# Attention diagonals and gate weights by small matmuls in a three-stage kernel

## The reference, cut to what matters

```
for t in range(S):
    cur = np.einsum('bhd,bhe->bhde', u[None] * kt, vt)
    y[:, :, t] = np.einsum('bhd,bhde->bhe', rt, state + cur)
    state = wt[:, :, :, None] * state + np.einsum('bhd,bhe->bhde', kt, vt)
```

## Time and profile before

| what | value |
|---|---|
| median of 3 runs | 981.27 us (980.72 to 982.27) |
| profiled execution, its own time | 980.96 us |
| its span, first to last instruction | 979.2 us |
| mean granted clock of TensorE | 0.992 |
| busy: PE, weight loads, DVE, ACT, POOL | 97%, 91%, 69%, 54%, 23% |
| first matmul of stage two (L786) | at 93.7 us of the span |

### The profile page before, as it was taken

One profiled execution on the slowest core, in us unless ns is written; L12 is line 12 of the kernel. 1 busy time (PEld: TensorE's weight loads), 2 busy tenths in 40 slices (PEclk: granted clock), 3 DMA queues, 4 the chain that ended last, 5 costly groups with the idle time before them and its releaser, 6 DMA issues.

```text
span 979.2 us, 18038 instructions
## 1 busy us (share of the span) xinstructions
PE 947.8 (97%) x6825; PEld 894.3 (91%) x6825; DVE 676.2 (69%) x1133; ACT 528.0 (54%) x986; POOL 222.8 (23%) x209
## 2 busy tenths in 40 slices
PE   6989999999999999999989999999999999999995
PEld 4656999999999999999989999999999999999995
DVE  6997769888888875437766765757767468565570
ACT  4454445454555544326545665756657467565560
POOL 0000000202020111021453233333243332334321
PEclk9999999999999999999999999999999999999998
DMA  9996343544445121126557887877968779787751
GB/s 346 302 320 184 115 142 116 160 150 129 134 143 163 50 71 38 51 67 234 188 161 191 237 278 233 250 235 220 307 205 247 254 207 292 218 242 256 200 156 17
DMA packets 94347, 183.74 MB, mean 188 GB/s; under 512 B 18274, under 2 KB 49764, under 8 KB 94260
## 3 DMA queue, kind: packets, MB, share of 16 engines
q1 hardware_dynamic: 80884, 161.90, 50.8%
q0 software_dynamic: 12976, 20.66, 10.2%
q10 hardware_dynamic: 400, 0.02, 0.0%
HBM read 156.94 MB, written 26.97 MB: 188 GB/s over the span
## 4 chain that ended last, share of the span: by engine, by line
PE 87%; DVE 5%; ACT 3%; issue 2%; DMA 1%; SPq 0%; another core or an unknown queue 0%; POOL 0%; DVEq 0%; ACTq 0%; POOLq 0%
PE pp L1231 20%; PE bank L1215 20%; PE bank L786 13%; PE bank L803 7%; PE fx L786 6%; PE fx L803 4%; PE yu L1274 3%; PE pp L184 3%; PE tr L1196 2%; PE yu L1256 1%; PE fx L1256 1%; PE yu L205 1%; PE yu L235 1%; PE tr L193 1%; DVE kdiv L263 1%
## 5 line engine op out<-in xcount | busy, mean ns | idle before, releaser
L1125 POOL DMA_INDIRECT result<-x2s,who x55 | 92.5, 1681 | 290.3 <-ACT x2s L1348 277.4
L1335 DVE SCALAR_TENSOR_TENSOR abl<-bank,abh 128x512 fp32r<-128x512 f32 x96 | 66.2, 691 | 113.7 <-ACT abh L1330 97.5
L976 POOL DMA_INDIRECT slot_entry<-entry,slot_i x48 | 52.1, 1086 | 334.7 <-DVE token_f L965 322.5
L1215 PE MATMUL bank<-xh,set_up_h 128*128 128x256 f32 x384 | 109.2, 284 | 0.0
L1215 PE MATMUL bank<-xh,set_up_l 128*128 128x256 f32 x384 | 108.6, 283 | 0.0
L1215 PE MATMUL bank<-xl,set_up_h 128*128 128x256 f32 x384 | 108.6, 283 | 0.0
L1330 ACT ACTIVATE abh<-bank 128x512 fp32r<-128x512 f32 x96 | 57.5, 599 | 85.1 <-PE bank L1215 79.6
L786 PE MATMUL bank<-xh,w12h 128*128 128x384 f32 x264 | 89.5, 339 | 1.0 <-DVE xl L483 0.9
L786 PE MATMUL bank<-xh,w12l 128*128 128x384 f32 x264 | 88.4, 335 | 0.0
L786 PE MATMUL bank<-xl,w12h 128*128 128x384 f32 x264 | 88.2, 334 | 0.0
L1231 PE MATMUL pp<-set_down_h,abh 128*128 128x384 f32 x256 | 87.7, 342 | 0.0
(11 more groups left out here) (254 smaller groups left out, 2641.4 us busy)
## 6 DMA issues: line engine op xcount, KB each, us to landing
up_raw<-in_moe_w SPq DMA_DIRECT2D x93, 512.0 KB
down_raw<-in_moe_w SPq DMA_DIRECT2D x124, 384.0 KB
wt<-in_w SPq DMA_DIRECT2D x16, 384.0 KB, 3.2
kt<-in_k SPq DMA_DIRECT2D x16, 384.0 KB, 3.1
rt<-in_r SPq DMA_DIRECT2D x16, 384.0 KB, 3.6
vs<-in_v_rows SPq DMA_DIRECT2D x16, 384.0 KB, 3.7
kn<-in_k_rows SPq DMA_DIRECT2D x16, 288.0 KB, 3.2
rn<-in_r_rows SPq DMA_DIRECT2D x16, 288.0 KB, 3.6
```

What stands on the lines that cost most here:

```text
L976: nc.gpsimd.indirect_dma_start(slot_entry, bass.IndirectOffsetOnAxis(slot_i[:, s, n:n + 1], 0), entry[:, s, n, :], None).then_inc(scattere ...
L1125: nc.gpsimd.indirect_dma_start(out, bass.IndirectOffsetOnAxis(who[v % 4][:, s, 0:1], 0), yo[v % 2][:, s, 0:DM], None, bounds_check=N - 1, ...
L1215: last = nc.tensor.matmul(bank[m % 2][:, f * T2:(f + 1) * T2], wp[:, kk, c:c + P], xp[:, kk, :], start=(n == 0), stop=(n == 3 * KD - 1))
L1335: nc.vector.scalar_tensor_tensor(hl[:, 2 * m:2 * m + 2, :].rearrange("p a t -> p (a t)"), bank[m % 2][:, :], 0.0, hh[:, 2 * m:2 * m + 2, : ...
```

## The change

For the pairs 0 to 4 (`by_matmul`, g <= 4) the diagonals come another way: one DVE instruction makes k*r*u with dimensions on partitions (`weighed`), six matmuls with a chunk of it as stationary operand and a 128 x 2 matrix of ones and zeros (`heads`) as moving one sum over each head, and ACT copies the 128 x 12 result. The second loads of k and r for these pairs go; `u` is also loaded in turned form (`u_side`), 16 bytes a partition. `ruk` and `added` have one buffer in place of two. A new load of kt or rt now also waits until the weighed product of the pair whose buffer it takes has been made.

The host sends w_out in both orders, so that the transpositions and their copies go and 1.5 MB (`woT`) is loaded in their place. The gates are made by 24 matmuls with blocks of woT as stationary and the 16 gate columns as moving operand. The first block of w3_mm is made without them, in the opening; its 16 columns follow as eight more matmuls (`gates_mm`), once DVE has written the gate columns.

```diff
-          "wo_turn": 2, "wo_gates": 5, "gates_turn": 1, "w3_mm": 5}
+          "wo_gates": 6, "gates_turn": 0, "gates_mm": 3, "w3_mm": 5}
...
+        def by_matmul(g):
+            return g <= HP
...
         def sp_input_load(sp, b, q, n):
             g, i = HP * b + q, q % 2
+            if n and by_matmul(g - 2):
+                need(sp, weighed_ready, g - 1)
...
         def dve_products(dve, b, q, part):
             g, i = HP * b + q, q % 2
-            if part == 0:
+            if by_matmul(g):
+                if part == 0:
+                    for n in (1, 2):
+                        dve.wait_ge(loaded[n][i], 16 * (2 * b + q // 2 + 1))
+                    dve.wait_ge(u_side_loaded, 16)
+                    need(dve, diag_full, g)
+                    nc.vector.scalar_tensor_tensor(weighed[:, :], rt[i][:, :], u_side[:, q:q + 1], kt[i][:, :],
+                                                   ALU.mult, ALU.mult).then_inc(weighed_ready, 1)
...
+        def pe_diag(pe, b, q):
+            g = HP * b + q
+            pe.wait_ge(weighed_ready, g + 1)
+            if g == 0:
+                pe.wait_ge(heads_ready, 4)
+            need(pe, diag_ready, g)
+            for c in range(NC):
+                last = nc.tensor.matmul(bank[0][:, 2 * c:2 * c + 2], weighed[:, c * C:(c + 1) * C], heads[:, :], start=True, stop=True)
+            last.then_inc(diag_full, 1)
...
+        def act_diag(act, b, q):
+            g = HP * b + q
+            act.wait_ge(diag_full, g + 1)
+            nc.scalar.copy(diag[:, :, :].rearrange("p c h -> p (c h)"), bank[0][:, 0:2 * NC]).then_inc(diag_ready, 1)
...
-            front = [("wo_turn", n, 0) for n in range(6)] + [("wo_gates", 0, 0), ("gates_turn", 0, 0)]
-            build = [("w3_mm", n, quarter) for n in range(KF) for quarter in range(4)]
+            front = [("w3_mm", 0, quarter) for quarter in range(4)]
+            build = [("wo_gates", 0, 0), ("gates_turn", 0, 0), ("gates_mm", 0, 0)]
+            build += [("w3_mm", n, quarter) for n in range(1, KF) for quarter in range(4)]
...
+                load_w3(0)
                 for n in (1, 2):
                     sp_input_load(sp, 0, 0, n)
-                load_w3(0)
-                sp_rows_load(sp, 0, 0)
-                sp.dma_start(u_all[:, :, :, :].rearrange("p q h d -> p (q h d)"),
-                             bass.AP(u.tensor, u.offset, [[0, P], [1, H * D]])).then_inc(small_loaded, 16)
+                sp.dma_start(u_side[:, :], u_turned[:, :]).then_inc(u_side_loaded, 16)
                 sp_values_load(sp, 0, 0)
+                sp.dma_start(woT[:, :, :], w_out_turned[:, :, :]).then_inc(woT_loaded, 16)
                 load_w3(1)
...
                     if step == "gates_turn":
-                        dve.wait_ge(gates_full, 2)
-                        nc.vector.tensor_copy(wo[:, :, DM:WA].rearrange("p (j t) e -> p t j e", t=2),
-                                              fx[:, 2 * P:4 * P].rearrange("p (t j e) -> p t j e", t=2, j=4)[:, :, :, 0:2 * E]
-                                              ).then_inc(wo_ready, 1)
+                        dve.wait_ge(gates_full, 1)
+                        nc.vector.tensor_copy(wo[:, :, DM:WA], gate_side).then_inc(wo_ready, 1)
...
+                    if step == "wo_gates":
+                        pe.wait_ge(woT_loaded, 16)
                         pe.wait_ge(gates_loaded, 16)
-                        pe.wait_ge(gates_clear, 1)
-                        for kk in range(KD):
-                            for n in range(4):
-                                last = nc.tensor.matmul(fx[4 * E * n:4 * E * (n + 1), 0:2 * P], gates[:, kk, :],
-                                                        woT[:, kk, 2 * P * n:2 * P * (n + 1)],
+                        pe.wait_ge(diag_ready, 1)
+                        for m in range(KF):
+                            for kk in range(KD):
+                                last = nc.tensor.matmul(gate_side[:, m, :], woT[:, kk, m * P:(m + 1) * P], gates[:, kk, :],
                                                         start=(kk == 0), stop=(kk == KD - 1))
                         last.then_inc(gates_full, 1)
...
+                    elif step == "gates_mm":
+                        pe.wait_ge(wo_ready, 1)
+                        for m in range(KF):
+                            last = nc.tensor.matmul(sums[0][:, DM:WA], w3T[0][:, m, :], wo[:, m, DM:WA],
+                                                    start=(m == 0), stop=(m == KF - 1))
+                        last.then_inc(wa_full, 1)
```

More of the change, by code:

```diff
@@ L55, in stands_alone, with program @@
     pool.sem_inc(waited, 1)
[L58 removed]
+def program(nc, w_turned, k_turned, r_turned, k_rows, r_rows, v_rows, u, u_turned, w1, w2, w3_turned, w_out, w_out_turned, gate_rows, noise_rows, ew1, ew2_rows, out):
     f32, f32r, i32 = mybir.dt.float32, mybir.dt.float32r, mybir.dt.int32
@@ L108, in program @@
         rdec = [asb(f"rdec{i}", [P, S]) for i in range(2)]
-        ruk = [asb(f"ruk{i}", [P, NC, 2, D]) for i in range(2)]
+        ruk = asb("ruk", [P, NC, 2, D])
+        weighed = asb("weighed", [P, S])
+        u_side, heads = asb("u_side", [P, HP]), asb("heads", [P, 2])
         kend_t = asb("kend_t", [P, NC - 1, P])
         att = asb("att", [P, 2, 2, 3, C])
-        added = [asb(f"added{i}", [P, NC - 1, D]) for i in range(2)]
+        added = asb("added", [P, NC - 1, D])
         state = [asb(f"state{i}", [P, NC - 1, HB]) for i in range(2)]
@@ L338, in act_products @@
             act.wait_ge(yu_full, 3 * g + 1)
-            nc.scalar.copy(added[q % 2][:, :, :], yu[:, 0:(NC - 1) * D].rearrange("p (c x) -> p c x", c=NC - 1)
+            nc.scalar.copy(added[:, :, :], yu[:, 0:(NC - 1) * D].rearrange("p (c x) -> p c x", c=NC - 1)
                            ).then_inc(yu_free, 1)
@@ L350, in act_state @@
                     act.wait_ge(yu_free, g + 1)
-                nc.scalar.activation(state[q % 2][:, c, 0:D], added[q % 2][:, c, :], ACT.Copy,
+                nc.scalar.activation(state[q % 2][:, c, 0:D], added[:, c, :], ACT.Copy,
                                      scale=decay[q % 2][:, c, C:C + 1]).then_inc(state_ready, 1)
@@ L410, in pe_attention @@
                 pe_output(pe, b, q, n)
+            elif step == "diag" and n == 1 and by_matmul(HP * b + q):
+                pe_diag(pe, b, q)
         def act_attention(act, b, step, q, n):
@@ L423, in act_attention @@
                 act_spread(act, b, q, n)
+            elif step == "diag" and n == 2 and by_matmul(HP * b + q):
+                act_diag(act, b, q)
             elif step == "keys":
@@ L574, in first_act @@
             def first_act(act):
-                nc.scalar.dma_start(gates[:, :, 0:2 * E], gate_rows[:, :, :]).then_inc(gates_loaded, 16)
-                def evacuate(n):
-                    act.wait_ge(wb_full, n + 1)
-                    nc.scalar.copy(woT[:, n % KD, (n // KD) * 512:(n // KD + 1) * 512], bank[n % 2][:, :]).then_inc(wb_free, 1)
+                nc.scalar.dma_start(gates[:, :, :], gate_rows[:, :, :]).then_inc(gates_loaded, 16)
                 for step, q, n in order:
                     act_attention(act, 0, step, q, n)
-                    if step == "wo_turn":
-                        evacuate(q)
-                    elif step == "wo_gates":
-                        act.wait_ge(gates_full, 1)
-                        nc.scalar.copy(gates_side[:, :], fx[:, 0:2 * P]).then_inc(gates_out, 1)
-                    elif step == "w3_mm" and n == 1 and 1 <= q <= 2 * KD:
+                    if step == "w3_mm" and n == 1 and 1 <= q <= 2 * KD:
                         m, kk = divmod(q - 1, KD)
@@ L593, in first_act @@
                         nc.scalar.copy(w12h[:, m, kk, :], wraw[(q - 1) % 2][:, :]).then_inc(w12h_ready, 1)
-                    elif step == "w3_mm" and n == 3:
+                    elif step == "gates_mm" or (step == "w3_mm" and n == 3 and q):
                         act.wait_ge(wa_full, q + 1)
@@ L615, in first_dve @@
                 nc.vector.memset(taken[:, :, :], 0.0)
+                for at in range(2):
+                    for h in range(2):
+                        nc.vector.memset(heads[at * HB:(at + 1) * HB, h:h + 1], float(at == h)).then_inc(heads_ready, 1)
                 for i in range(2):
@@ L676, in first_pe @@
                             pe.wait_ge(w3_loaded[q % 2], 16 * (q // 2 + 1))
-                            pe.wait_ge(wo_ready, 1)
                             need(pe, wal_ready, q - 1)
+                        if q == 0 and n % 2 == 0:
+                            pe.wait_ge(wo_loaded[n // 2], 16)
+                        columns = slice(0, WA if q else DM)
                         for m in range(2 * n, 2 * n + 2):
-                            last = nc.tensor.matmul(sums[q % 2][:, 0:WA], w3T[q % 2][:, m, :], wo[:, m, :],
+                            last = nc.tensor.matmul(sums[q % 2][:, columns], w3T[q % 2][:, m, :], wo[:, m, columns],
```

(2 more changed lines are left out.)

64 lines of the change are left out of this document (26 added, 38 removed).

## The result

The changed kernel takes 995.93 us (median of 4 runs, 994.56 to 997.21) against 981.77 us for the kernel before (4 runs, 980.72 to 984.39): 14.2 us slower, a ratio of 1.0141 (95% interval 1.0125 to 1.0156). Forecast were 988.2 us. The profiled execution took 994.56 us, with a span of 992.6 us.

A forecast was written before the change was run, and what follows sets the result against it. TensorE was taken to become the bound before stage two, delays reaching the end one for one. Opening 3.6, added work 7.0, old waits -6.5, new waits 6.0, low clock -3.1: +7.0 us, forecast 988.2 us, range 981.0 to 993.0.

The forecast's parts named there:

- TensorE as the bound: Up to stage two TensorE becomes the bound over VectorE; a later start of stage two reaches the end one for one.
- the price of a small matmul: Added matmuls with full stationary blocks and 2 or 16 moving columns: 0.11 us an instruction.
- the wait for the copy: Before gates_mm, TensorE waits for VectorE's copy of the gate columns behind pair 0's state chain: 1.95 us.
- the second halves: Pairs 1 and 2: the second half of the scores waits for VectorE's mask, 0.5 us each.
- The sum without a fall of the clock: All terms before stage two, no new low clock: first stage-two matmul near 100.7 us, +7.0 us in all.
- the opening: Work ahead of pair 0's scores: block 0's quarters and diagonals; scores start at 18.35 us, 3.6 us later.
- with the loss at the low clock gone and none new: Before stage two: the 3.1 us lost to TensorE at 1.2 GHz vanish and no new such loss comes.
- The rival: TensorE's clock falls during the gates, doubling part of them and the next block: +4 us, 992.2 us; chance 15%.
- the stretch behind it as long as before: From the start of stage two on: matmuls untouched, duration unchanged, so no added time there.
- the half pace: TensorE's slow start: the first 4 us of new work run at half pace, 2 us more.
- The new waits: TensorE's added waits before stage two, for the gate copy, scaled states, masks and xl: together 6.0 us.
- the wait of the output behind ACT: Pair 0: ACT scales states behind its cast of block 0, so the output waits about 0.9 us.

The follow-up runs named there:

- the wide ones: Changed kernel with each gate matmul's moving operand widened from 16 to 96 columns, 80 of them zeros: 990.37 us, ratio 1.009 to the kernel before.
- the third group: Later runs on one chip; its unaltered kernel before, profiled there as reference, took 978.41 us, ratio 1.0.
- the old roles: Gate operands changed back, 32 gate columns stationary, 256 woT columns moving: ratio 1.0026 for the gates' part against the kernel before; whole change, early copy, 168 bytes padding, 0.9999.

## Why the prediction was wrong, by its own steps

**Right.** TensorE as the bound and one for one through the first 329 us of stage two; the price of a small matmul, 0.11 us: 48 gate matmuls took 5.50 us as against 5.3 where the clock stayed at the full level (the wide ones), and twelve diagonals 1.40 against 1.3; the first w3T at 10.28 us as against 9.9; the wait for the copy, 1.87 us as against 1.95; the second halves, two waits of 0.5 us as against 0.5 each; xl, 1.2 as against 1.4; the old waits for keys gone; `weighed` at 1.0 us as against 0.95. The sum without a fall of the clock gave a start at 100.7 us, and the kernel whose clock stayed up through the gates started at 100.73. That closeness is partly luck: the opening was 1.1 us too small and the waits 1.1 us too large, as shown below, and that kernel still had a short fall.

The Trainium skill, page "TensorE: Matmul & The Clock Gate", section "Back-to-back issue gap", has about 81 ns for a weight load and matmul of a sustained stream at 128 columns; at that figure the 48 gates would take 3.9 us, an estimate. The traces do not agree for full fp32 blocks: 5.4 us from the first of the 48 to the one behind them, 0.113 us each, at the full clock.

**Wrong: "with the loss at the low clock gone and none new".** This step of the sum failed. The loss before was 3.1 us; the new kernel ran for some 13.7 us at 1.2 GHz. By the rows at either level: gates 6.05 in place of 5.50, scores 1.65 in place of 0.94, state 1.31 in place of 0.79, gates_mm 3.60 in place of 1.96, four quarter matmuls 3.01 in place of 1.5. These are 0.6 + 0.7 + 0.5 + 1.6 + 1.5 = 4.9 us. Widening the moving operand took away 4.2 us of the start.

The rival was named and given 15%. My argument against it was that the gates follow one another without a pause. The trace shows them without a pause and the clock falling all the same: a full PE column in the windows is no cover against it. The windows of the kernel with 96 moving columns are about as full there (weight loads 5.91 of 6.00 us), and its clock did not fall. The rival's price of 4 us was right; its total of 992.2 us was 3.7 us low, 2.2 of them by the next point.

**Wrong: "the stretch behind it as long as before".** No instruction there was changed, and I took that for proof that none would run slower. But the change makes the attention's buffers 128 bytes a partition smaller, and what is allotted behind them moves down. The down matmuls of stage three then have records of 338 in place of 334 to 335 ns. Records of pipelined matmuls are no pace, so the stretch is the measure: 2.2 us, of which 1.9 came back with 40 unused bytes, against kernels without padding on other chips (884.1 us). Chips differ too: the unchanged kernel has 885.50 us in the first profile and 881.9 in the third group. The changed place costs about 2.2 us against either.

**Smaller terms.** The opening was sized 1.1 us too small: the scores began at 19.41, not 18.35 us. The first load landed 0.4 us late, and the twelve matmuls ahead of the diagonals took some 6.4 us by their starts: up to 15.3 us they follow 0.64 us apart, behind it 0.32. So the half pace lasted 5 us and not the 4 us of the sum, though the windows print a clock of 1.00 there. The new waits were 1.9 + 1.2 + 1.0 + 0.8 = 4.9 us in place of 6.0; the wait of the output behind ACT did not appear. With the 4.9 us of the rows at the low clock this makes 7.0 + 1.1 + 4.9 - 1.1 = 11.9 us, where 11.2 were measured; the 0.7 us I have not placed. With 2.2 us behind, the spans differ by 13.4 us; the last 0.8 us up to the difference of the medians lie between executions.

**Parts of the change.** The gates' part costs 12.4 us by itself, almost all through its operand roles and the wait that it makes. The diagonals' part by itself moves the start by nothing that the falls of the clock do not cover (92.16 to 94.71 us without padding, against 93.17 and 93.70 for the kernel before), and costs 2.2 us by layout (ratios 1.0025, 1.0026 and 1.003, and 0.9991 with 40 unused bytes). Together they start stage two 2.1 us earlier than the gates alone (104.94 against 107.03), though they bring more matmuls. The gates alone waited longer, but they also ran at the low clock for some 27 us in place of 13.7; how the 2.1 us divide was not taken apart.

**Open.** Why 128 bytes lower is slow was not tried, nor which of the moved buffers does it; no kernel with the diagonals' part had its later buffers exactly where the kernel before has them. The narrow operand is shown to bring the long fall; what in it the clock answers to is not. Why the clock fell at 24 us with the old roles in the two kernels without the diagonals' part, and not in the three with it, is open too.

## What to carry to other kernels

For a product with one narrow operand, make the narrow one stationary and let several such blocks run side by side: 24 instructions with 32-wide blocks, four at a time, took 1.5 us, 48 with full blocks 5.5 to 8.5 us. With full fp32 blocks they stood 0.11 us apart at the full clock whether 16 or 96 columns moved. A row of such loads can look 100% busy and still let the clock fall, and then it is the work behind that pays double; look at the granted clock before calling an added block cheap. When later stages with untouched instructions change by a few nanoseconds an instruction, compare buffer addresses, and try some unused bytes before looking further. Read the addresses from the built program; adding up sizes missed the rounding here.

## What the runs showed that I had not expected

Zeros can pay: 80 more moving columns in 48 matmuls left them 0.11 us apart and made the kernel 4.6 us faster. And a shift of the buffers by 128 bytes a partition costs 2.2 us in matmuls that start some 390 us behind the part that was changed; 40 bytes of padding, a shift of 64, return it.
